# Moving the v cast to GpSimd, reordering the token-id work, and loading the first w1 whole, in a fused attention and expert kernel

## The reference

```
expert_idx = token_ids * 2654435761 % 8        # the low three bits of the id decide
for e in range(8):
    xe = x[expert_idx == e]
    out[expert_idx == e] = max(xe @ w1[e], 0) @ w2[e]     # 512 -> 1024 -> 512
```

## Time and profile before

| | |
|---|---|
| three runs | 226.3, 227.34, 227.33 us; median 227.33 |
| the profiled execution | 226.3 us, span 224.6 us, granted TensorE clock 1.00 |
| busy over the span | PE 86%, DVE 56%, POOL 54%, ACT 47% |
| DMA | 54.96 MB, mean 245 GB/s |

### The profile page before, as it was taken

One profiled execution on the slowest core, in us unless ns is written; L12 is line 12 of the kernel. 1 busy time (PEld: TensorE's weight loads), 2 busy tenths in 40 slices (PEclk: granted clock), 3 DMA queues, 4 the chain that ended last, 5 costly groups with the idle time before them and its releaser, 6 DMA issues.

```text
span 224.6 us, 4635 instructions
## 1 busy us (share of the span) xinstructions
PE 193.6 (86%) x1786; PEld 130.8 (58%) x1788; DVE 126.0 (56%) x276; ACT 106.4 (47%) x133; POOL 120.4 (54%) x226
## 2 busy tenths in 40 slices
PE   0529976967777799999989999999999999999991
PEld 0328665856565667774654854854855845845640
DVE  5777999988898975899932412412421422412220
ACT  3447887888878837673521331331322322322411
POOL 6600658887996999910005857806715615126053
PEclk9999999999999999999999999999999999999999
DMA  5999999999999999999995599999799799113023
GB/s 144 400 392 393 388 390 390 391 391 395 387 390 392 281 176 186 204 210 206 210 208 157 146 191 228 357 192 237 200 207 258 143 206 228 73 40 147 26 93 134
DMA packets 29791, 54.96 MB, mean 245 GB/s; under 512 B 2367, under 2 KB 11583, under 8 KB 29760
## 3 DMA queue, kind: packets, MB, share of 16 engines
q0 software_dynamic: 16544, 26.22, 56.2%
q1 hardware_dynamic: 13216, 28.35, 34.3%
HBM read 61.90 MB, written 10.49 MB: 322 GB/s over the span
## 4 chain that ended last, share of the span: by engine, by line
PE 49%; DVE 21%; DMA 15%; SPq 9%; issue 3%; ACT 1%; POOL 1%; DVEq 0%; POOLq 0%
PE ps L721 26%; PE ps L695 20%; SPq L495 8%; DMA kf<-in_k_dram 7%; DMA vf<-in_v_dram 7%; DVE selA L477 3%; DVE xn L596 3%; DVE vx L514 1%; DMA tok<-in_moe_token_ids_dram 1%; DVE xT L653 1%; DVE oneh L609 1%; DVE selB L465 1%; DVE zz L433 1%; DVE selB L468 1%; ACT ek L509 1%
## 5 line engine op out<-in xcount | busy, mean ns | idle before, releaser
L739 POOL DMA_INDIRECT out_dram<-yo,idx x40 | 39.5, 988 | 75.5 <-ACT yo L731 55.4
L721 PE MATMUL ps<-w2b,hT 128*128 128x512 bf16 x320 | 70.4, 379 | 0.0
L695 PE MATMUL ps<-xT,w1b 128*128 128x320 bf16 (+1 forms) x512 | 64.4, 286 | 0.3 <-DVE xn L596 0.3
L695 PEld LDWEIGHTS ps<-xT,w1b 128*128 128x128 bf16 x512 | 49.8, 98 | 14.5 <-DVE xn L596 0.7
L721 PEld LDWEIGHTS ps<-w2b,hT 128*128 128x128 bf16 x320 | 31.3, 98 | 36.2
L653 POOL COPY xT<-xs x112 | 45.0, 455 | 9.3 <-issue 2.3
L702 ACT ACTIVATE hT<-ps 128x640 bf16<-128x640 f32 x41 | 28.8, 703 | 36.2 <-PE ps L695 35.9
L731 ACT ACTIVATE yo<-ps 128x512 f32<-128x512 f32 x26 | 15.5, 597 | 55.2 <-PE ps L721 55.2
L704 DVE TENSOR_SCALAR hT<-ps 128x640 bf16<-128x640 f32 x23 | 19.0, 824 | 30.2 <-PE ps L695 30.2
L733 DVE COPY yo<-ps 128x512 f32<-128x512 f32 x14 | 9.7, 692 | 44.0 <-PE ps L721 44.0
L619 PE MATMUL ps<-oneh,xn 128*128 128x384 bf16 (+1 forms) x160 | 22.8, 297 | 3.9 <-DVE xn L596 3.9
(11 more groups left out here) (105 smaller groups left out, 139.1 us busy)
## 6 DMA issues: line engine op xcount, KB each, us to landing
qf<-in_q_dram SPq DMA_DIRECT2D x8, 1152.0 KB, 15.5
kf<-in_k_dram SPq DMA_DIRECT2D x8, 1152.0 KB, 15.7
w2b<-in_moe_w_dram POOLq DMA_DIRECT2D x16, 512.0 KB, 11.7
vf<-in_v_dram SPq DMA_DIRECT2D x7, 1152.0 KB, 15.4
w1b<-in_moe_w_dram POOLq DMA_DIRECT2D x14, 512.0 KB, 8.4
vf<-in_v_dram SPq DMA_DIRECT2D x2, 576.0 KB, 14.7
w1b<-in_moe_w_dram POOLq DMA_DIRECT2D x4, 256.0 KB, 6.0
out_dram<-yo,idx POOLq DMA_INDIRECT x40, 3.8
```

Of the source, the lines that this page charges most:

```text
L695: em.op("pe", [lambda e, d=d, k=k: e.matmul(cut(PB[:, u + k, 0:H2]), w1b[s][:, d, 128 * (f + k):128 * (f + k) + 128], cut(rhs(d)), start=( ...
L721: em.op("pe", [lambda e, fc=fc: e.matmul(PB[:, u, :], hT[hp][:, fc, 128 * t:128 * t + 128], w2b[s][:, fc, :], start=(fc == 0), stop=(fc == ...
L739: em.dma("pool", "d_o%d" % y, lambda e: e.indirect_dma_start(out=out[:, :], out_offset=IndirectOffsetOnAxis(ap=idx[:, 5 * ee + t:5 * ee + ...
```

## The change

- The token ids are loaded from ACT's queue instead of SP's, where they stood ahead of all loads.
- The PE sums and the seven DVE operations that make `pos` move into a function `positions()`, called behind the transposes of batch 0.
- `one_hot(0)` and `one_hot(7)` move from before the loop to behind the attention of batch 0 and of batch 1.
- `cast_v` runs on POOL. The halved cast of batch 7 (`cast_half`) stays on DVE.
- The first clearing of `xT` on POOL no longer waits for the flags.
- Expert 0's w1 comes in one piece, two DMAs, that wait for the k of batch 7; the second pair of expert-0 tiles (`l1(0, 2)`) moves behind the sort of batch 7, and the PSUM banks change with it.

```diff
-    em.dma("sync", "d_tok", lambda e: e.dma_start(
+    em.dma("act", "d_tok", lambda e: e.dma_start(
         tok64[:], moe_token_ids.rearrange("(b p c) -> p b c", b=B, p=64, c=NC)), P=[b_tok])
...
-    em.op("pe", [lambda e: e.matmul(TOT, ones[:], flg2, start=True, stop=True),
...
+    def positions():
+        em.op("pe", [lambda e: e.matmul(TOT, ones[:], flg2, start=True, stop=True),
+                     lambda e: e.matmul(CUM, upper[:], flg2, start=True, stop=True)],
+              R=[b_flg, bc["upper"], bc["ones"]], W=[bk[6], bk[7]])
+        dv(lambda e: e.tensor_copy(out=tots[:], in_=TOT), R=[bk[7]], W=[b_tots])
...
     def cast_v(p):
-        dv(lambda e: e.tensor_copy(out=vx[p][:, :, :, 0:DH], in_=vf[p][:]), R=[b_v[p]], W=[b_vx[p]])
+        gp(lambda e: e.tensor_copy(out=vx[p][:, :, :, 0:DH], in_=vf[p][:]), R=[b_v[p]], W=[b_vx[p]])
...
-            gp(lambda e, g=g: e.memset(v[:, g, :, H2 + SEG[0]:CAP].bitcast(F32), 0.0), P=[b_xT], R=[b_flg])
+            gp(lambda e, g=g: e.memset(v[:, g, :, H2 + SEG[0]:CAP].bitcast(F32), 0.0), P=[b_xT])
...
-    one_hot(0)
-    one_hot(B - 1)
     for b in range(B):
         p = b % 2
         exp_k(p)
         transpose_q(p)
-        if b > 0:
+        if b == 0:
+            positions()
+        else:
             sort(b - 1, 0, 3, 5)
...
-            first_weights()
+            weights1(0, 0, R=[b_k[1]])
             segments(b - 1, (1,))
...
         attend(p, 4, 1, 5)
+        if b < 2:
+            one_hot((0, B - 1)[b])
         if b == 0:
             segment_table()
             widths()
...
     l1(0, 0, 0, 3, True)
-    l1(0, 2, 0, 0, True)
...
-    sort(B - 1, 0, 3, 5)
+    sort(B - 1, 0, 0, 5)
     sort(B - 1, 2, 6, 2)
...
-    for i, (ee, f) in enumerate([(0, f) for f in range(4, FC, 2)] + [(1, f) for f in range(0, FC, 2)]):
-        l1(ee, f, 0, (0, 3, 6)[i % 3], True)
+    for i, (ee, f) in enumerate([(0, f) for f in range(2, FC, 2)] + [(1, f) for f in range(0, FC, 2)]):
+        l1(ee, f, 0, (3, 0, 6)[i % 3], True)
```

More of the change, by code:

```diff
@@ L337, in fused_kernel @@
     CUM, TOT = PB[:, 6, 0:NF], PB[:, 7, 0:NF]
-    em.op("pe", [lambda e: e.matmul(TOT, ones[:], flg2, start=True, stop=True),
-                 lambda e: e.matmul(CUM, upper[:], flg2, start=True, stop=True)],
-          R=[b_flg, bc["upper"], bc["ones"]], W=[bk[6], bk[7]])
     b_tots, b_sx, b_cs, b_pr, b_pos = Buf(), Buf(), Buf(), Buf(), Buf()
@@ L345, in fused_kernel @@
     gb = gbase[:].rearrange("p b g -> p (b g)")
[L346 to L356, removed]
+    def positions():
[3 more added lines that the diff above has]
+        dv(lambda e: e.tensor_copy(out=tots[:], in_=TOT), R=[bk[7]], W=[b_tots])
+        dv(lambda e: e.tensor_tensor_scan(out=fl(sx), data0=tots[:], data1=tots[:], initial=0.0, op0=ALU.add,
+                                          op1=ALU.bypass), R=[b_tots], W=[b_sx])
+        dv(lambda e: e.tensor_tensor(out=fl(sx), in0=fl(sx), in1=tots[:], op=ALU.subtract), R=[b_tots], W=[b_sx])
+        dv(lambda e: e.tensor_tensor(out=fl(cs), in0=CUM, in1=fl(sx), op=ALU.add), R=[bk[6], b_sx], W=[b_cs])
+        dv(lambda e: e.scalar_tensor_tensor(out=fl(prod), in0=fl(cs), scalar=1.0, in1=flg2, op0=ALU.add,
+                                            op1=ALU.mult), R=[b_cs, b_flg], W=[b_pr])
+        dv(lambda e: e.tensor_reduce(out=pos[:], in_=prod[:].rearrange("p b e t -> p b t e"), axis=AX.X, op=ALU.add),
+           R=[b_pr], W=[b_pos])
+        dv(lambda e: e.tensor_tensor(out=pos[:], in0=pos[:], in1=gb.unsqueeze(2).to_broadcast([128, NG, TG]),
+                                     op=ALU.subtract), R=[bc["gbase"]], W=[b_pos])
     def segment_table():
@@ L670, in weights1 @@
                 W=([b_w1[s]] if a == 0 else ()), P=(() if a == 0 else [b_w1[s]]))
[L672 to L682, removed]
     def weights2(ee, s):
@@ L689, in weights2, with layer1 @@
                 W=([b_w2[s]] if a == 0 else ()), P=(() if a == 0 else [b_w2[s]]))
-    def layer1(s, f, hf, rhs, bx, hp, u, onact, ee=None, bw=None):
+    def layer1(s, f, hf, rhs, bx, hp, u, onact, ee=None):
         def cut(ap):
@@ L697, in layer1 @@
             cut(rhs(d)), start=(d == 0), stop=(d == 3))
-            for k in range(2) for d in range(4)], R=[bw or b_w1[s]] + bx, W=bk[u:u + 2])
+            for k in range(2) for d in range(4)], R=[b_w1[s]] + bx, W=bk[u:u + 2])
         o = hT[hp][:, f:f + 2, H2 * hf:H2 * hf + H2]
@@ L714, in l1 @@
         layer1(ee % NW, f, hf, lambda d: xT[:, d, CAPS * ee + H2 * hf:CAPS * ee + H2 * hf + H2],
-               [b_xT] if hf == 0 else [b_xT, b_x6, b_x7], ee % 2, u, onact, ee if hf else None,
-               b_wf[f // (FC // 2)] if ee == 0 else None)
+               [b_xT] if hf == 0 else [b_xT, b_x6, b_x7], ee % 2, u, onact, ee if hf else None)
     def layer2(s, t, hp):
@@ L844, in index_table @@
            R=[b_idf, b_ov8], W=[b_idx])
-    for i, (ee, f) in enumerate([(0, f) for f in range(4, FC, 2)] + [(1, f) for f in range(0, FC, 2)]):
-        l1(ee, f, 0, (0, 3, 6)[i % 3], True)
+    for i, (ee, f) in enumerate([(0, f) for f in range(2, FC, 2)] + [(1, f) for f in range(0, FC, 2)]):
+        l1(ee, f, 0, (3, 0, 6)[i % 3], True)
     for f in range(0, FC, 2):
         l1(0, f, 1, lslot(), True)
-    b_w1[0] = Buf(*b_wf)
     for ee in range(E):
```

## The result

The changed kernel took 233.77 us (median of 4 runs, 233.43 to 234.18) against 227.32 us: a ratio of 1.0296, 95% interval 1.0261 to 1.0331. I had forecast 231.3 us, slower. The profiled execution took 234.02 us, span 232.3 us.

What follows compares the result with a forecast made beforehand. Loads pace attention and set the first expert matmul's start; then PE runs almost without pause. Lateness 5.9 - 0.2 - 0.9 - 0.3 = +4.5 on 226.3 gives 230.8, forecast 231.3; main case 229 to 234, range 227.2 to 237.5 us.

Steps and rivals of the forecast that it cites:

- The price of the cast: On POOL, casting v of one batch (2304 elements) takes 2.1 us, reckoned from POOL's copies.
- The upper end of 4.1 us: Slow-cast rival: POOL's cast of v takes 4.1 us, as its own small casts suggest, giving 239.6 us; chance 15%.
- The token ids: On SP's queue, loads behind the ids land 0.5 us earlier (0 to 0.8), counting only while loads set the pace.
- The queue behind the tables: On POOL, cast(1) waits behind the tables and runs 29.5 to 31.6 us; kv(1) starts at 31.7 instead of 26.09.
- kv(1) to kv(2): On PE, DVE and ACT, one batch from kv to the end of its sort takes 8.3 us, putting kv(2) at 40.0.
- The steps after it: In attention, kv(2) at 40.0 us and kv(6) at 76.3, 5.9 us late against the kernel before.
- the recurrence: Cast ends 8.0 us after the previous cast or xs of two batches back; kv follows cast or previous kv plus 8.3.
- The two-batch loop (c): On POOL, segments wait for xs, ready 9.5 us after that batch's kv, and the cast two batches on stands behind them.
- the slices of the DMA would fall below 390 GB/s: Sign that the forecast is right: DMA slices fall below 390 GB/s before 73 us.
- w1 hidden by 0.9 us: At the first expert matmul, expert 0's w1 lands at 87.2 us against a start at 88.1, so PE does not wait.
- the rival of the late w1: At the first expert matmul, the whole w1 lands 1.5 to 2 us later than reckoned and PE stands; 233 us, 10%.
- The wait for `selA`: Ahead of the index table, PE's 0.9 us wait goes, as DVE's chain moves 4.4 us, less than PE's 5.7.

Runs made afterwards that it cites:

- number 2: The kernel before with only v of batches 0 to 6 cast by POOL; 233.61 us, ratio 1.0259.
- 9: The kernel before with v of batches 0, 1 and 2 cast by POOL one step ahead, batches 3 to 6 on DVE; 227.82 us, ratio 1.0048.
- number 7: The kernel before with v of batches 0 to 6 cast by POOL, each cast after the first one step earlier on its queue; 235.09 us, ratio 1.0307.
- 4: The changed kernel with 26 matmuls that nobody reads added on PE ahead of kv(1); 234.86 us, ratio 1.0326.
- 5: The changed kernel with one_hot(7) moved right behind one_hot(1); 235.24 us, ratio 1.0311.
- number 6: The changed kernel with 26 unread matmuls on PE ahead of kv(1) and one_hot(7) right behind one_hot(1); 233.15 us, ratio 1.0237.
- number 3: The changed kernel with cast(1) put ahead of the segment tables on POOL's queue; 234.26 us, ratio 1.0295.

## Why the prediction was right, and where its terms were off

The price of the cast: 2.1 us predicted; 2.11 to 2.14 us in six of the seven casts, 15.1 us in all, 2.35 us where DVE's position chain ran beside cast(0). The upper end of 4.1 us and the factor of 2 were too high; against DVE's 1.36 us it is 1.55.

The token ids: 0.5 us predicted for the loads. Cast(0), which waits for v 0, started at 12.76 us against 13.61 in number 2, which has the old queue (13.89 and 14.03 in 9 and 7): at least 0.85 us. As predicted, nothing of it was left at batch 6.

The queue behind the tables: cast(1) predicted at 29.5, kv(1) at 31.7; measured 29.51 and 31.76, with the tables free of DVE's cast lock (0.65 us for the operation that took 1.52).

kv(1) to kv(2) is the term that was mis-sized: 8.3 us predicted, 11.0 measured, and that is the whole miss at kv(6) (78.67 for 76.3). I took 8.3 from a stretch in which the clock was 1.00 and PE had not stood idle, and I charged `one_hot(7)` 1.1 us on the scaling of batch 2, where it falls on the sort of batch 1 through a PSUM bank. Numbers 4, 5 and 6 show both and that either is enough to hold kv(2) near 42; with both gone the step is 8.43.

The steps after it: 36.3 us predicted from kv(2) to kv(6), 36.0 measured. That they agree so well is in part luck. My 36.3 had the 1.1 us of `one_hot(7)` in it, which fell before kv(2); without it the recurrence gives 35.2, which is what number 6 measured at full clock, and some 0.8 us of the 36.0 is the second dent of the clock. The two-batch loop (c) is seen in POOL's waits for `xs` of 3.85 and 1.94 us; so POOL was not busy without a gap, as I had written. That the slices of the DMA would fall below 390 GB/s was wrong too: up to the last loads enough were queued to hide the late releases (v took a median of 10.0 us from issue to landing, 15.4 before), and that sign would have misled a reader. The loss appears behind them, in the two slices at 33 and 62 GB/s.

From kv(6) on: w1 hidden by 0.9 us predicted, 0.76 us of waiting measured, so that cover was 1.7 us short. The issue came 4.1 us behind kv(6) and not 3.4, as POOL waited 1.07 us for `xs` of batch 5, and the first tile could start 8.25 us after the issue, not 7.5. This is the rival of the late w1, in part: as late as it said, with 0.76 us of waiting. The wait for `selA` went as predicted. In sum +4.5 predicted and +7.7 in the two profiled executions: 2.4 at kv(2), 0.8 at w1.

The mechanism was right: kv waits for casts that queue on POOL behind the tables and the segments, and the loop through `xs` lets nothing be made good. I let its start hang on the place of cast(1); number 3 mends that place and loses as much at the lower clock, number 7 brings the casts forward and the segments are late instead.

What I had wrong beside it is how full POOL was. The earlier trace rows reads 60 to 100% from 34 to 73 us, not 80 to 100, and the stretch of the earlier trace rows holds 22 copies, more than the 16 of a batch; the three stretches of 9 us ahead of it read 7.41, 7.78 and 7.79 us. The copies of a batch took 5.6 to 6.9 us before, part of it lost to DVE's casts. With the cast it is 5.6 + 2.1, some 7.8 us, still 1.2 less than the loads need for a batch. The loss is in what stands behind what on the queue, and in what each of them waits for; that POOL had no room for the casts is not shown.

The forecast was 231.3 us, and 233.77 lies near the top of its 229 to 234.

Still open: what makes the clock fall a second time in the changed kernel (0.65 and 0.50 over 54 to 58 us, PE busy 1.02 us of 50 to 52), and whether some order of POOL's queue holds all seven casts without a loss.

## What to carry to other kernels

Before moving work to another engine, list what the moved instruction will stand behind on its new queue, what will stand behind it, and what each of them waits for. The busy time alone does not tell: with the cast POOL had 7.8 us of work in a batch of 9, and yet in each order of the seven casts kv, the segments or w1 came late. Follow the loop that this closes: when one round through the queue takes about as long as the pace of the loads, a late start is never made good. When one step is late for one reason, look for the next that would hold it as long: here the slow clock and a PSUM bank each hid the other, and only the kernel with both taken away showed the sum. A small transfer that went out first and alone landed 2.7 us after its issue; from another queue and together with large loads it took 8.5 us. No run tells the company from the queue.

## What the runs showed of the hardware that I had not expected

What DVE loses beside POOL's cast is more than the copies had shown: in the changed kernel a subtraction of two SBUF tiles took 2.27 us instead of 0.56 beside cast(0), and five one-hots took up to 3.31 us instead of 1.12 beside a cast and the copies behind it (3.64 in number 7):

```profile
13.25 2.27 DVE L351 TENSOR_TENSOR sx<-sx,tots 128x384 f32<-128x384 f32 x1
49.45 3.31 DVE L611 TENSOR_SCALAR oneh<-col,pos 128x384 bf16<-128x384 f16 x5
```

The column of the granted clock does not tell all: kv(0) takes 2.13 us in the changed kernel, as kv(1) does at 0.50, in a stretch whose column reads 1.00 (the third number from the end). The kernel before has the same 2.13 us at 15.44. The length of like matmuls is the surer sign.

```profile
15.21 2.13 PE L548 MATMUL ps<-vx,ek 64*128 64x130 bf16 x36 [3.59 <-POOL vx L516]
14.00:23.00 9.00, 7.00 (x94) 6.47 (x94) 8.07 (x14) 4.57 (x4) 1.11 (x1) 1.00 1.06 392
```
